# A fused attention and two-layer-pair MLP kernel on one core: transposed tiles in single PSUM banks, softmax inverses spread through DRAM, first weight tiles split on POOL, and a new start

## The reference, cut to what matters

```python
batch, n_heads, seq, head_dim = (4, 8, 576, 64)          # q, k, v: float32
q_rot, k_rot = (rotate(q), rotate(k))                     # rotary embedding, halves of 32
scores = scale * np.matmul(q_rot, k_rot.transpose(0, 1, 3, 2))
scores = scores - np.max(scores, axis=-1, keepdims=True)
attn = np.exp(scores)
attn = attn / (np.sum(attn, axis=-1, keepdims=True) + 1e-09)
x = np.matmul(attn, v)                                    # -> transposed and reshaped to [2304, 512]
h = x @ w_in                                              # [512, 2048]
r = np.maximum(h, 0.0)
x = (s * (r * r) + b) @ w_out                             # [2048, 512]
h = x @ w2_in
g = h * (1.0 / (1.0 + np.exp(-1.702 * h)))
return g @ w2_out
```

## Time and profile before

| | us |
|---|---|
| median of 3 runs | 1165.56 (1165.14 to 1165.83) |
| the profiled execution | 1168.41 |
| its span | 1166.6 |
| start to the first score matmul | 20.57 |
| passes 1 to 14 | 50.82 to about 334.9, 20.29 each |
| last H and Y work of the MLPs | from 355.48 to the end |
| PE busy | 1112.1 of 1166.6 |

### The profile page before, as it was taken

How to read it: one execution, slowest core, us unless ns; L and a number is a source line. 1 busy time by engine, 2 the same in 40 slices (tenths; PEclk the granted TensorE clock), 3 DMA queues, 4 the chain that set the end, 5 groups by cost and what they waited for, 6 DMA issues and landing times.

```text
span 1166.6 us, 17049 instructions
## 1 busy us (share of the span) xinstructions
PE 1112.1 (95%) x6608; PEld 1049.9 (90%) x6608; DVE 547.9 (47%) x889; ACT 512.6 (44%) x1013; POOL 238.1 (20%) x254
## 2 busy tenths in 40 slices
PE   3899999999988999999999999999999999999998
PEld 3788888888888999999999999999999999999997
DVE  3777778777765643333333335643233333323222
ACT  2777777787763542233232325542222222222222
POOL 6776867778331000000000000000000000000000
PEclk9999999999998999999999999999999999999999
DMA  6555655545313320000000003400000000000000
GB/s 137 126 122 111 142 131 122 119 111 124 72 26 103 126 71 1 1 1 1 1 1 1 1 1 98 128 29 1 28 1 15 14 1 28 1 28 1 28 1 28
DMA packets 95985, 60.60 MB, mean 52 GB/s; under 512 B 62624, under 2 KB 83232, under 8 KB 95904
## 3 DMA queue, kind: packets, MB, share of 16 engines
q1 hardware_dynamic: 95008, 59.01, 20.3%
q10 hardware_dynamic: 896, 0.49, 0.1%
HBM read 31.16 MB, written 4.72 MB: 31 GB/s over the span
## 4 chain that ended last, share of the span: by engine, by line
PE 91%; ACT 3%; issue 2%; DVE 2%; DMA 1%; POOL 1%; SPq 1%; ACTq 0%; POOLq 0%
PE psum L756 34%; PE psum L728 34%; PE psum L514 8%; PE psum L449 4%; PE psum L480 4%; PE psum L477 2%; PE psum L464 1%; PE psum L536 1%; ACT ET L560 1%; ACT QK L583 1%; DVE QK L656 1%; PE psum L526 1%; PE psum L496 1%; PE psum L534 0%; DMA wraw<-in_moe_w_out_dram 0%
## 5 line engine op out<-in xcount | busy, mean ns | idle before, releaser
L728 PE MATMUL psum<-xhi,Whi 128*128 128x384 f32 x768 | 258.5, 337 | 4.7 <-DVE Wlo L221 4.7
L728 PE MATMUL psum<-xhi,Wlo 128*128 128x384 f32 x768 | 258.4, 336 | 0.0
L728 PE MATMUL psum<-xlo,Whi 128*128 128x384 f32 x768 | 257.8, 336 | 0.0
L728 PEld LDWEIGHTS psum<-xhi,Whi 128*128 128x128 f32 x768 | 144.7, 188 | 9.2 <-DVE Wlo L221 5.0
L728 PEld LDWEIGHTS psum<-xlo,Whi 128*128 128x128 f32 x768 | 144.7, 188 | 4.1
L728 PEld LDWEIGHTS psum<-xhi,Wlo 128*128 128x128 f32 x768 | 144.6, 188 | 0.0
L885 DVE SCALAR_TENSOR_TENSOR glo<-act,sb_sb,ghi 128x384 fp32r<-128x384 f32 x96 | 59.7, 622 | 147.3 <-ACT ghi L862 147.3
L862 ACT ACTIVATE ghi<-act,sb_sb 128x384 fp32r<-128x384 f32 x96 | 59.2, 617 | 157.5 <-PE psum L756 153.6
L756 PE MATMUL psum<-ghi,Whi 128*128 128x384 f32 x384 | 128.3, 334 | 0.0
L756 PE MATMUL psum<-glo,Whi 128*128 128x384 f32 x384 | 128.3, 334 | 0.0
L756 PE MATMUL psum<-ghi,Wlo 128*128 128x384 f32 x384 | 128.3, 334 | 0.0
(11 more groups left out here) (92 smaller groups left out, 1855.9 us busy)
## 6 DMA issues: line engine op xcount, KB each, us to landing
Q<-QK SPq DMA_DIRECT2D x64, 144.0 KB, 2.5
QK<-QK SPq DMA_DIRECT2D x32, 288.0 KB, 3.3
wraw<-in_moe_w_in_dram SPq DMA_DIRECT2D x32, 256.0 KB, 2.8
wraw<-in_moe_w_out_dram SPq DMA_DIRECT2D x32, 256.0 KB, 3.1
rest<-O SPq DMA_DIRECT2D x32, 144.0 KB, 2.3
raw<-in_q_dram SPq DMA_DIRECT2D x32, 128.0 KB, 3.0
raw<-in_k_dram SPq DMA_DIRECT2D x32, 128.0 KB, 2.5
vraw<-in_v_dram SPq DMA_DIRECT2D x32, 128.0 KB, 2.4
```

Of the source, the lines that this page charges most:

```text
L728: mm = pe.matmul(hps(n), w[i][:, kt * P:(kt + 1) * P], x[C % 2][:, kt, :], start=kt == 0 and j == 0, stop=kt == KT - 1 and j == 2)
```

## The change

- **X tiles in single banks.** `X` transposes only its four `E` tiles (512 columns, one bank); the four tail blocks that rode on them go to a new job `XQ`, four transposes in one bank, read by `hiQ` and `loQ`. `XT` is as before. `freed` now works by banks, so that two X jobs share what was one slot. `Xhi` and `Xlo` hold both heads.
- **Inverses through DRAM.** `widen` and `B` go. `IT` transposes the nine inverses (one transpose), ACT copies the 9x128 result (`icp`), SP writes it to DRAM (`put`) and three DMAs read it back, repeated over 64 rows (`get`). `finish` moves to POOL, as one multiply of 128x576.
- **The halves of PV.** `evac` copies only 64 rows; `sum` on DVE adds the other 64 rows straight from PSUM. The DMA `rest` and POOL's `add` go. Both heads now have the same column layout, which costs two more small matmuls in the second head's PV.
- **W.** POOL splits tiles 0 and 1 after passes 13 and 14 (`first_w`); tiles 2 and 3 are loaded after passes 14 and 15; ACT and DVE split tile 2 when the last PV is done, and run one tile further ahead in the first chunk.
- **Start.** DVE rotates both heads of pair 0, POOL waits for that. ACT issues q's and k's copies of head 0 of pair 0, each q part as soon as it is there.
- **All five orders and the bank list are new.**

```diff
-    PE_ORDER = order("S12@0 prep0@2 S13@0 X00@0 X01@0 S00@1 S01@1 ST@1 prep1@2 S02@1 S03@1 X02@0 X03@0 S10@1 PV1@-1 "
-                     "X10@0 X11@0 XT@0 X12@0 X13@0 B@-1 S11@1 PV0@0")
+    PE_ORDER = order("XQ@-1 XT@-1 IT@-1 X10@-1 X11@-1 X12@-1 X13@-1 S00@1 PV0@-1 S01@1 prep0@2 X00@0 X01@0 S02@1 "
+                     "prep1@2 S03@1 S10@1 S11@1 S12@1 ST@1 X02@0 X03@0 S13@1 PV1@-1")
+    ACT_ORDER = order("hi03@-1 exp13@0 expT@0 evac1@-2 hiQ@-1 hiT@-1 icp@-1 hi10@-1 hi11@-1 hi12@-1 hi13@-1 exp00@1 "
+                      "evac0@-1 qk0@2 hi00@0 exp01@1 hi01@0 qk1@2 exp02@1 exp03@1 exp10@1 exp11@1 exp12@1 hi02@0")
+    DVE_ORDER = order("klo0@2 lo00@0 max02@1 lo01@0 max03@1 klo1@2 max10@1 max11@1 max12@1 maxT@1 max13@1 lo02@0 lo03@0 "
+                      "sum1@-1 loQ@0 loT@0 lo10@0 lo11@0 lo12@0 max00@2 lo13@0 inv@1 max01@2 sum0@0")
+    POOL_ORDER = order("finish@-3 vlo1@-1 rot1@2 V0@0 vlo0@0 rot0@3 V1@0")
+    SP_ORDER = order("put@-1 load0@3 qcopy0@2 load1@3 loadv1@0 kcopy0@2 loadv0@1 get@-2 qcopy1@2 kcopy1@2")
+    SLOTS = [7, 2, 6, 0, 1, 3, 2, 3, 2, 0, 1, 7, 6, 2, 1, 0, 3, 2, 1, 0, 7, 6, 2, 1]
+    BANK_ORDER = (7, 6, 0, 1, 4, 5, 2, 3)
...
+        def first_w(pool, s, zero):
+            i = s - (NPAIR - 3)
+            if 0 <= i < AHEAD:
...
+                pool.tensor_tensor(Whi[i][:], wraw[:, i, :], zero[:, :].broadcast_to([P, 2 * DM]), ALU.add).then_inc(w_hi_done, 1)
+                split_w(pool, i, False)
...
+                def put_inv(p, _, __):
+                    sp.wait_ge(invT_copied, p + 1)
+                    need(sp, inv_in[p % 2], 48 * (p // 2))
+                    sp.dma_start(inv_dram[p % 2], invT[p % 2][:]).then_inc(inv_out[p % 2], 16)
+
+                def get_inv(p, _, __):
+                    sp.wait_ge(inv_out[p % 2], 16 * (p // 2 + 1))
+                    need(sp, x_done, p)
+                    flat = inv_dram[p % 2].rearrange("t p -> (t p)")
+                    for h, at, a, n in ((0, 0, 0, S), (1, 0, S + TAIL, MAIN), (1, MAIN, S, TAIL)):
+                        sp.dma_start(inv_row[rows_of(h), at:at + n],
+                                     flat[a:a + n].rearrange("(o q) -> o q", o=1).to_broadcast([D, n])).then_inc(inv_in[p % 2], 16)
...
+                    if s in (NPAIR - 2, NPAIR - 1):
+                        load_weights(sp, s - NPAIR + 4)
...
+                def finish(p, _, __):
+                    b, t = p // KT * S, p % KT
+                    pool.wait_ge(sum_done, 2 * p + 2)
+                    pool.wait_ge(inv_in[p % 2], 48 * (p // 2 + 1))
+                    pool.tensor_tensor(xT[:, t, b:b + S], osum[p % 2][:], inv_row[:], ALU.mult).then_inc(x_done, 1)
...
+                def XQ_job(p, _, __):
...
+                    for j in range(NM):
+                        mm = pe.transpose(ps[:, j * P:(j + 1) * P], ET[p % 2][:, j * P:(j + 1) * P], id_sb[:])
+                    mm.then_inc(xQ_t, 1)
...
+                    act.copy(O[r, :], row(banks("PV", h), 0)[r, :]).then_inc(evac_done, 1)
...
+                def total(p, h, _):
+                    dve.wait_ge(evac_done, 2 * p + h + 1)
+                    if h == 0:
+                        need(dve, x_done, p - 1)
+                    r = rows_of(h)
+                    dve.tensor_tensor(osum[p % 2][r, :], row(banks("PV", h), 0)[rows_of(1 - h), :], O[r, :], ALU.add).then_inc(sum_done, 1)
...
+                    if p == 0 and h == 0:
+                        act.wait_ge(qk_hi, 1)
+                        q_copy(act, p, h, 0)
+                        act.wait_ge(qk_lo, 1)
+                        q_copy(act, p, h, 1)
+                    elif p == 0:
+                        k_copy(act, 0, 0)
```

## The result

The changed kernel's median is 1131.87 us (1131.05 to 1132.98, 4 runs) against 1165.69 for the kernel before (1165.14 to 1167.19, 4 runs): a ratio of 0.9708, with a 95% interval of 0.9692 to 0.9725. Forecast was 1131.0. The profiled execution took 1132.01, its span 1130.2, against 1168.41 and 1166.6. The trace before is of an execution 2.7 us above its median (granted clock 0.994, where those near the median have 0.996 or 0.997), the one after of one 0.1 above, so the medians are 33.8 us apart and the spans 36.4.

What follows compares the result with a forecast made beforehand. PE's work and its round trips through ACT and DVE bound attention, PE alone the MLPs. Start -7.1, passes -18.1 and -3.0, MLPs -6.4, together -34.6, gave 1131.0 us against the median 1165.56; range 1116 to 1147.

Steps and rivals of the forecast that it cites:

- start: Kernel start: earlier rotation and copies bring pass 1 to 43.7 us, before 50.82; gain 7.1 us.
- passes 1 to 13: Steady attention passes: 18.9 us each, 13 times 1.4 less, -18.1 us.
- passes 14 to 16: Last attention passes, with W split by POOL: 37.9 us for 40.9, -3.0 us.
- MLPs: First MLP steps: the wait for W tile 2 and matmuls at the lower clock go, -6.4 us.
- The walk: One changed pass followed job by job from XQ, with each bank's last reader: 16.63 us of work, 1.55 of waits.
- the 1.55 of the half-rotation: At the start, DVE's second half-rotation took 1.55 us beside POOL's byc; if it came back, the start would be 1.05 later.
- surcharges: Added to the pass: 0.3 us for PV0 and 0.2 for PV1 for waits on many semaphores, four refills about 0.06 each.
- refills: PE after a wait: the first work runs longer, about 0.06 us each, four a pass, an estimate.
- second rival: Attention passes: round trips stay, `sum0` on DVE a new wait; 19.7 to 20.3 us a pass, 1142 to 1151; chance 0.20.
- the prediction's line: SP's queue in a pass: needs 16.2 + 3x us with its waits, x the issue price of each `get`.
- SP as the bound: Attention passes: SP's issues set the pass, slower than before with x above 1.73; near 1.6, 1160; chance 0.06.
- The first rival: Attention passes: the waits nearly vanish, 17.7 us a pass, 1114 us; chance 0.12.

Runs made afterwards that it cites:

- E1: Changed kernel with the old start: POOL rotates head 1 of pair 0, SP issues all q and k copies; 1131.92 us against 1131.87.
- E7: Changed kernel with DVE rotating both heads of pair 1 too, POOL starting with pair 2; 1131.18 us against 1131.87.
- E9: Changed kernel with all handling of W as before: ACT and DVE split tiles 0 and 1, tiles 2 and 3 load after attention; 1142.18 us.
- E5: Changed kernel with the first tile of each X job transposed twice, eight more transposes a pass; 1140.15 us against 1131.87.
- E10: Changed kernel with five transposes in each X job and four more ahead of the inverses' transpose; 1147.68 us against 1131.87.
- E3: Changed kernel with each `sum` done twice on DVE, the first time into a tile nobody reads; 1150.12 us against 1131.87.
- E6: Changed kernel with each `sum` done twice and `inv` moved ahead of `sum1` in DVE's order; 1150.35 us against 1131.87.
- E8: Changed kernel with each `get` done three times, two of them to tiles nobody reads; 1167.91 us against 1131.87.
- E2: Changed kernel with W tiles 2 and 3 loaded after attention and tile 2 split in the first chunk; 1137.36 us against 1131.87.
- E4: Changed kernel with `inv` moved ahead of `sum1` in DVE's order, from behind `lo13`; 1133.2 us against 1131.87.
- E12: Changed kernel with `inv` early, `sum0` ahead of max01 and pair 1 rotated on DVE; 1131.63 us against 1131.87.
- E11: Changed kernel with six more transposes a pass, all in X00 and X01, where PE has gaps; 1131.65 us against 1131.87.

## Why the prediction was right, point by point

**The total** was 0.9 off: the medians fell 33.8 for the 34.6 of the sum. The terms, though, are read from the two traces, whose spans fell 36.4, and there the sum is 1.8 too small. Two things make the total better than its terms, and both are luck: the errors of single terms have both signs, and the trace before was of an execution 2.7 above its median. At which of its waits that execution lost more than others, no trace shows.

| term | forecast | measured, by the terms' own marks | by a job that both orders share |
|---|---|---|---|
| start | -7.1 | -6.15 | +0.2 |
| passes 1 to 13 | -18.1 | -21.8 | -20.2 (12 passes) |
| passes 14 to 16 | -3.0 | -2.1 | -9.9 |
| MLPs | -6.4 | -6.4 | -6.4 |

**The start: the step that failed.** The walk began a pass after at XQ and compared it with the earlier trace rows and pass 1 of before, which begins at prep0. These are different jobs: the new order puts XQ earlier in the same work. By these marks the term came out, -6.15 for -7.1, but it is not a gain of the start. By a job that both have, prep0 of pair 3, before is at 51.19 and after at 51.37. The early first S (forecast 18.5, measured 18.61) came true and is worth nothing, as E1 shows by 0.05 us. If the 1.55 of the half-rotation was worth anything, E1 does not show it, as it did not come back there. What comes next is pair 1: I put the end of its first rotation at 18.5 for 19.53; it ended at 19.9, because its last load was issued at 11.73 and landed 3.22 later, and POOL could not begin before 15.1. With POOL out of it (E7) IT comes 0.7 earlier and 0.7 us are gained at best. The shared job moves the missing 7 into the row of passes 14 to 16: from prep0 of pair 15 to H0 it is 50.7 for 60.6. E9, with W handled as before, takes 58.7 there, so 8.0 of these 9.9 are W's.

**The pass: right in kind, 0.3 too long.** The walk without surcharges gives 18.18: 12.53 for the stretch from S12 to S01 and 5.65 for the rest. Counted from start to start, as the walk counts, the trace has 12.67 from S12 to prep0 (169.14 to 181.81) and 5.90 from there to the next S12. The waits in the walk were S02 0.23, prep1 0.21, S10 0.76 and S12 0.35; by starts they measure 0.39, 0.41, 0.79 and 0.28, with the refills in them. So PE waited where the walk said, and the pass is 0.4 longer than the walk in all, refills included. The surcharges were 0.74. The 0.5 in them for waits on several semaphores ahead of the PVs does not exist: PV0 starts right behind S00. The refills exist and are a little dearer than the 0.06 each that I estimated: by starts S12 takes 0.65 for 0.53. The term that failed in size is thus the 0.5. Thirteen times 0.3 is 3.9, which is most of -21.8 for -18.1.

**Where a pass's 1.7 us come from.** The net of the transposes is eight fewer. Put back in X (E5) they cost 0.65, so that much is shown to be PE's work taken out of its unbroken stretch. The other 1.06 is fewer waits with their refills: 20.29 less 17.4 of work leaves 2.9 before, 18.58 less 16.6 leaves 2.0 after. The new orders and the freed banks bring this together. No experiment takes them apart, since the old orders do not fit the new banks; that stays open. E10, with four transposes more than before, still has a pass 0.6 shorter, so that the waits fell is shown; which of the edits did it is not. Over the kernel, E5 puts 8.3 us on the transposes and E9 10.3 on W; if they add up, about 15 of the 33.8 are these waits.

**`sum` and the second rival.** `sum` costs 756 ns, as forecast, not 1450. The rival's mechanism is real: with two adds of 1.43 together (E3) the kernel takes 1150.1, inside the 1142 to 1151 that the rival gave for 1.45, and E6 shows its second part too, `sum1` holding X12.

**The inverses' trip.** Hidden, as forecast, with `get` three times in 1.82, x = 0.61, so by the prediction's line SP needs 16.2 + 1.8 = 18.0 with its waits, under 18.58. The 16.2 is not worked out there, and the trace shows more room: in passes 1 to 12 SP stands idle 0.7 to 3.4 us ahead of head 0's q copies, 2.0 on the mean, waiting for `klo0`. With three times as many (E8) x is about 1.85, 0.62 for each single issue on the mean, the line gives 21.7, and 21.2 was measured, with single issues stretched. So SP as the bound is a real mechanism and the line near its size; the rival failed on the price. That the kernel then takes as long as before, close to the deciding point x = 1.73, is in part luck, as 8.8 of the 36 us come behind the passes.

**W.** Forecast were 6.4 in the MLPs and 3.0 in the last passes; E9 gives 10.3 for all of it and E2 5.5 for the late tile alone. The lower clock, the wait and the slower PV of the earlier trace rows come back in them.

**The first rival,** passes of 17.7, would need PE's gaps gone. E4, E12 and E11 show why they stay: they are DVE's eight jobs from max01 to `klo1`, done between PE's S01 and S12, and neither a lighter DVE ahead of them nor PE work beside them changes this.

## What to carry to other kernels

Compare two orders of one loop by a job that both have, not by where each is said to begin. In a loop that two engines share, find the part in which each of them never waits: six transposes cost 0.65 us in PE's unbroken stretch and nothing in its gaps. A walk that names each bank's last reader found the right waits here, and the surcharge added for semaphores was its largest error within a pass. When an experiment costs as much as the forecast says, look where the time went: a quarter of E8's did not lie in the loop.

## What the runs showed of the hardware

A DVE operation of nine columns can last as long as a POOL operation beside it. In order of time after, and then all 16 of them (ns, shortest, median and longest):

```profile
309.77 1.42 POOL L460 TENSOR_TENSOR xT<-osum,inv_row 128x576 f32<-128x576 f32 x1
309.83 1.38 DVE L685 TENSOR_TENSOR sums_eps<-sums,eps 128x9 f32<-128x9 f32 x1
...
L685 DVE TENSOR_TENSOR sums_eps<-sums,eps x16: 158/652/1384, 32.5 to 309.8; 128x9 f32<-128x9 f32 x16
```

The two times that no POOL operation lies beside it, it takes 158 and 160 ns; the other 14 times it ends within 0.04 us of one of POOL's. The Trainium skill, "SBUF — State Buffer", section "Who interferes with whom", says that a DVE instruction with two SBUF inputs contends with a GpSimd one that reads SBUF; the trace agrees, and adds that even nine columns wait to the end of the other's instruction. The pass of 18.92 is the one in which it took 1.12.

SP's issues are not of one price: the same `get` took 0.60 by itself and a pair of them 2.40, when SP issued nearly without a break (E8).
